# Attention, a mixer with an MLP, and a gated MLP on one core: weight splitting moved between engines and stages, and the element lists of the second product redrawn

## The chip, the cores and the metric

One core of one Trainium2 chip. The metric is the time of one execution on the device in microseconds; the median of the runs is used. Lower is better.

## What is computed

Three layers in a row, all in fp32, with batch 4, 576 positions and width 512.

```python
# attention: 8 heads of 64, window 128, a linear bias per head
scores = q @ k.T / 8 + bias;  attn = softmax(where(0 <= i - j < 128, scores, -1e9));  x = attn @ v
# "Moe": a mixer of rank 32 over positions, then an MLP 512 -> 2048 -> 512
u  = x + ((x.T @ U) @ V).T
x2 = u + maximum(u @ w_ch1, 0) @ w_ch2
# "Moe2": 512 -> 1024, half of it normalised and mixed over positions, a gate, and 512 -> 512
h = maximum(x2 @ w_in, 0);  a, v = h[..., :512], h[..., 512:]
v = w_spatial @ layernorm(v) + b_spatial
out = (a * v) @ w_out
```

## The kernel before

**Precision.** Every large fp32 product is done as three products of split numbers: each operand x is stored as a high part (a copy in the type fp32r) and a low part (x minus the high part, fp32r as well), and TensorE adds high x high, low x high and high x low in PSUM. So each operand needs a copy (in most places on ScalarE) and a subtraction (on VectorE or GpSimd).

**Seven products.** The two MLP products of Moe, `up` (512 -> 2048) and `down` (2048 -> 512), are each done in a block scheme in which seven half-sized products stand in for eight. It needs sums and differences of the four blocks of each operand (names A11, A12, A22, S1 to S4 on the side of the weights, m = 1 to 7 for the products).

**Stages on TensorE**, in order of time: attention with the mixer (16 pairs of heads; a step per pair, steps of the last batch overlap the start of `up`), `up` (24 units s = 0..23, that is 3 groups g of tokens by 8 pairs of columns u; a unit is 7 products of 6 matmuls of 384 columns), `down` (3 groups by 7 products by 8 entries kk of 6 matmuls of 384 columns), Moe2 (4 batches, each `half_v`, `half_u`, `spatial`, `output`).

**Order.** Each engine runs one instruction list written out by hand, with counting semaphores between them. All DMAs are issued by SyncE from one list. A wait in any list holds everything behind it in that list. The parts that matter here:

- In attention GpSimd makes the low parts of the attention output (`lo_x`, L656) and the split of the first unit of w_ch1 (`first_w1`, L691 to L703), and at its end sums and low parts of the first group of u (`x_sum`, `lo_xs`, L665 to L682). VectorE's reads of PSUM, scores (L1167), copies (L1176) and denominators (`sums`, L1183 to L1186) are steps of the same chain. SyncE loads q/k and v two pairs ahead at most (`load_qk`, `load_v`, L375 and L382).
- In `up` ScalarE keeps three partial results per unit (`keep_p`, L934), writes one block (`c21`), VectorE adds the others (`c11` L1368, `c12` L1374, `relu_b` L1380, `c22` L1386), and SyncE stores the four blocks of a unit to DRAM, r_scr (`store_r`, L421). The staging tile has two halves, so the additions of unit s wait for the store of unit s-2. `keep_p(s, 7)` must be done before the product (s, 4).
- w_ch2 is split during `up`, one of its 8 parts kk at a time, in the units that `W2_UNIT = {9: 0, 10: 1, 11: 2, 12: 3, 13: 4, 14: 5, 17: 6, 18: 7}` names: VectorE forms four sums (L1344 to L1349), ScalarE the high parts (`w2_shi_of` L925, `w2_hi_of` L918 and L919; L925 waits until all six stores of the part before have landed), VectorE the low parts (L1353, L1329, L1331), SyncE stores them (`store_w2`, L440 to L443, six DMAs) and they are read back in seven pieces of 2 MB (`load_w2q`, L447).
- In `down` the relu'd blocks a, b, c, d come back (`load_raw`, L451). `raw_c` lies in memory that `up` uses to its end. Each entry is one kk: ScalarE writes its high part (`hi_r`, L953), VectorE its low part (`lo_r`, L1393, L1396), in a ring of `RING = 5` tiles of 384 columns. Sums of blocks (`r_sum`, L1405, L1410, L1415, L1419) are made in halves of 1536 columns, and the list puts `r_sum(0, 3, 0)` right behind the fourth entry of the first product. `add_res` (L1429) and `dc` (L1439, L1446) add the residual and the partial results.
- Moe2's weights (17 parts: 4 of w_in's v half, 4 of its u half, 4 of w_out, 5 of w_spatial) are loaded into the four slots of `w1raw` (`load_wc`, L502 and L503) and split in the last group of `down` and behind it: ScalarE `hi_wc` (L982, L984), GpSimd `lo_wc` (L710). The high parts of the v half come behind entry 0 of product (2, 2), those of the u half together with `hi_x2` (L994) behind entry 1 of (2, 4), those of w_out in (2, 3), and those of w_spatial behind the last entry, in front of `relu_v(0)` (L1081), which frees the PSUM tile of `half_v` (L1805).

## Time and profile before

| | |
|---|---|
| median of 3 runs | 808.46 us (808.29 to 809.04) |
| the profiled execution | 811.25 us, span 809.5 us |
| attention until the first product of `up` | 0 to about 150 us of the span |
| `up` | to about 376 us |
| `down` | to 587.03 us |
| Moe2 | to the end |

The boundaries are read from the first and last matmuls of each part. Parts overlap a little: two tail steps of attention run among the first units of `up`. "Busy" counts a matmul from its start to its modelled end, and matmuls overlap; where the text counts matmuls in a stretch, the product of count and pace tells more than the busy time.

### The profile page before, as it was taken

The numbers are of one execution on the slowest core, as the hardware profiler recorded it, in microseconds if no ns is written. First come the engines' busy times: TensorE is split into PE (matmuls) and PEld (weight loads), VectorE is DVE, ScalarE is ACT, GpSimd is POOL, SyncE is SP. The second block draws the span as 40 slices with busy tenths as digits, with TensorE's granted clock in tenths as the row PEclk, the third lists the DMA queues.
The fourth block names the chain that finished last, engine by engine and source line by source line (L and its number), as shares of the span: only waits on it lengthen the run. The fifth ranks groups of instructions, "written<-read, shape, count | busy, mean of one in ns | idle before, by whom it ended". The sixth has DMA issues, their size and how long they took to land.

```text
span 809.5 us, 13413 instructions
## 1 busy us (share of the span) xinstructions
PE 739.8 (91%) x4688; PEld 678.3 (84%) x4688; DVE 491.4 (61%) x1149; ACT 377.8 (47%) x889; POOL 97.5 (12%) x77
## 2 busy tenths in 40 slices
PE   8999999889998788895589999979879999999998
PEld 5777777789997778894589989969869899899998
DVE  6877787877675566321586896795827436416422
ACT  5977787635443343322235455536535233342322
POOL 1611136700000000000000000121331010000100
PEclk9999999999999899898779999999999999999999
DMA  6433242345368876599855625623460010000101
GB/s 205 124 110 103 88 152 73 130 156 183 120 234 279 284 241 206 192 384 421 313 183 191 195 77 197 246 65 121 131 247 1 1 60 1 25 34 0 58 0 59
DMA packets 74547, 119.20 MB, mean 147 GB/s; under 512 B 4992, under 2 KB 56704, under 8 KB 73600
## 3 DMA queue, kind: packets, MB, share of 16 engines
q1 hardware_dynamic: 74496, 118.55, 42.7%
q8 instruction: 29, 0.48, 0.2%
q14 instruction: 22, 0.18, 0.1%
HBM read 70.82 MB, written 47.71 MB: 146 GB/s over the span
## 4 chain that ended last, share of the span: by engine, by line
PE 70%; DVE 10%; DMA 10%; issue 4%; SPq 3%; ACT 3%; POOL 0%; DVEq 0%; ACTq 0%
PE bank L1840 4%; PE bank L1841 4%; PE bank L1842 4%; PE bank L1682 4%; PE wide L1697 3%; PE bank L1878 3%; PE bank L1880 3%; PE bank L1879 3%; PE bank L1989 2%; PE bank L1664 2%; DMA w_scr<-tok 2%; PE bank L1991 2%; PE bank L1990 2%; PE bank L1807 2%; PE bank L1805 2%
## 5 line engine op out<-in xcount | busy, mean ns | idle before, releaser
L1840 PE MATMUL bank<-xs,w1s 128*128 128x384 f32 x336 | 118.7, 353 | 20.0 <-ACT sums_u L934 15.8
L953 ACT ACTIVATE rk<-tok 128x384 fp32r<-128x384 f32 x144 | 73.6, 525 | 97.5 <-PE wide L1880 48.7
L1841 PE MATMUL bank<-xs,w1s 128*128 128x384 f32 x336 | 116.7, 347 | 0.0
L1842 PE MATMUL bank<-xs,w1s 128*128 128x384 f32 x336 | 116.5, 347 | 0.0
L1878 PE MATMUL bank<-rk,w2q 128*128 128x384 f32 x208 | 73.1, 351 | 32.0 <-DVE rk L1393 28.3
L1840 PEld LDWEIGHTS bank<-xs,w1s 128*128 128x128 f32 x336 | 66.4, 198 | 24.4 <-ACT sums_u L934 18.3
L796 ACT ACTIVATE sc<-sc,mn 128x256 f32<-128x256 f32 (+1 forms) x144 | 67.0, 468 | 20.7 <-DVE mn L1167 20.6
L934 ACT ACTIVATE sums_u<-bank 128x384 f32<-128x384 f32 x72 | 35.2, 489 | 83.0 <-PE bank L1842 80.0
L1878 PEld LDWEIGHTS bank<-rk,w2q 128*128 128x128 f32 x208 | 40.2, 193 | 37.5 <-DVE rk L1393 30.5
L1880 PE MATMUL bank<-rk,w2q 128*128 128x384 f32 x208 | 71.1, 342 | 0.0
L1879 PE MATMUL bank<-rk,w2q 128*128 128x384 f32 x208 | 71.1, 342 | 0.0
L1841 PEld LDWEIGHTS bank<-xs,w1s 128*128 128x128 f32 x336 | 66.6, 198 | 0.0
L1842 PEld LDWEIGHTS bank<-xs,w1s 128*128 128x128 f32 x336 | 66.4, 198 | 0.0
L1396 DVE TENSOR_TENSOR rk<-tok,rk 128x384 fp32r<-128x384 f32 x96 | 51.0, 564 | 23.0 <-ACT rk L953 23.0
L710 POOL TENSOR_TENSOR wvl<-w1raw,wvh 128x512 fp32r<-128x512 f32 x4 | 7.5, 1896 | 362.8 <-ACT wvh L984 362.8
L1167 DVE CUSTOM_DVE_ANT_0 sc<-bank,bias 128x256 f32<-128x256 f32 (+1 forms) x128 | 42.3, 384 | 5.4 <-PE bank L1644 3.5
L1176 DVE COPY pt<-bank 128x512 f32<-128x512 f32 x48 | 31.4, 682 | 20.8 <-PE bank L1682 20.8
L1878 PE MATMUL wide<-rk,w2q 128*128 128x384 f32 x128 | 43.3, 338 | 0.6 <-DVE rk L1396 0.5
L1880 PE MATMUL wide<-rk,w2q 128*128 128x384 f32 x128 | 43.0, 336 | 0.0
L1879 PE MATMUL wide<-rk,w2q 128*128 128x384 f32 x128 | 43.0, 336 | 0.0
L1879 PEld LDWEIGHTS bank<-rk,w2q 128*128 128x128 f32 x208 | 40.3, 194 | 0.0
L1880 PEld LDWEIGHTS bank<-rk,w2q 128*128 128x128 f32 x208 | 40.2, 193 | 0.0
(222 smaller groups left out, 1830.7 us busy)
## 6 DMA issues: line engine op xcount, KB each, us to landing
r_scr<-tok SPq DMA_DIRECT2D x19, 768.0 KB, 4.1
w2q<-w_scr SPq DMA_DIRECT2D x7, 2048.0 KB, 14.5
tok<-r_scr SPq DMA_DIRECT2D x18, 768.0 KB, 5.8
qkraw<-qk SPq DMA_DIRECT2D x32, 288.0 KB, 3.0
w1raw<-w SPq DMA_DIRECT2D x32, 256.0 KB, 3.7
w_scr<-tok SPq DMA_DIRECT2D x12, 512.0 KB, 3.5
u_scr<-tok SPq DMA_DIRECT2D x6, 768.0 KB, 4.6
raw_c<-r_scr SPq DMA_DIRECT2D x6, 768.0 KB, 4.6
```

The lines of the kernel that those rows point to most:

```text
L796: act.activation(w, w, ACT.Exp, bias=mn[:, s, n:n + 1], scale=-1.0, accum_out=sm[:, i, c:c + 1]).then_inc(exp_done, 1)
L934: act.activation(sums_u[:, i, :], a_ps[s % 2][:, 0:HT], ACT.Copy).then_inc(kept, 1)
L953: act.activation(rk[:, n % RING, 0], raw[RAW_OF[m]][:, kk, :], ACT.Relu if m <= 3 else ACT.Copy).then_inc(rk_hi, 1)
L1167: dve.tensor_tensor_reduce(out=out, in0=src, in1=add, scale=-SCALE, scalar=3e38, op0=ALU.add, op1=ALU.min, accum_out=mn[:, s, n:n + 1]).th ...
L1396: dve.tensor_tensor(lo, x, hi, ALU.subtract).then_inc(rk_lo, 1)
L1682: last = pe.transpose(pt_ps[f % 2][:, j * P:(j + 1) * P], sc[:, i % 2, n, w * P:(w + 1) * P], ident[:, :])
L1840: pe.matmul(o, wh, ah, start=(k == 0 and m in FRESH), stop=False, skip_group_check=True)
L1841: pe.matmul(o, wl, ah, start=False, stop=False, skip_group_check=True)
L1842: last = pe.matmul(o, wh, al, start=False, stop=(k == 1), skip_group_check=True)
L1878: pe.matmul(o, wh, rh, start=(kk == 0 and m in FRESH), stop=False, skip_group_check=True)
L1879: pe.matmul(o, wl, rh, start=False, stop=False, skip_group_check=True)
L1880: last = pe.matmul(o, wh, rl, start=False, stop=(kk == UNITS - 1), skip_group_check=True)
```

## The change

It has four parts.

1. **Moe2's weights.** SyncE loads the 17 parts in attention into nine slots of a new tile `wprep` (at the place where `xs` lies later), GpSimd makes both the high part (`tensor_copy`) and the low part (in place), SyncE stores them to a new DRAM tensor `wc_scr`. The tables WC_AFTER, WC_LOAD and WC_STORE say at which pair. They are read back as finished pairs near the end of `down` (`load_group`), and `hi_wc`, `lo_wc` are gone. SyncE's and GpSimd's attention loops are unrolled.
2. **w_ch2.** The sums and the low parts are GpSimd's (`split_w2`), the high parts stay with ScalarE, later in the unit (behind `keep_p(s, 6)`), and wait for the stores of the six blocks' classes separately (`w2_out_t` for A11, A12, A22; `w2_out_s` for S1 to S4). W2_UNIT becomes 9, 10, 11, 12, 13, 15, 16, 18.
3. **`down`'s lists.** An entry is a pair of kk (768 columns), `RING` is 3 such entries, sums are made in quarters at places that FIRST_T and NEXT_T name, the last unit of `up` already makes the first three high parts, the loads are ordered anew, `raw_c`, `late`, `u_in` and the `w2q` tiles have other places.
4. **Small moves.** The low parts of m = 7, 5, 4 of the first group of u go from GpSimd to VectorE; the last four mixer products (`mix_up`) are spread over units 1 to 4 where three of them stood in unit 2; stores of u follow at unit 5.

```diff
-RING = 5
+RING = 3
+DP = UNITS // 2
+SLOTS = 9
-W2_UNIT = {9: 0, 10: 1, 11: 2, 12: 3, 13: 4, 14: 5, 17: 6, 18: 7}
+W2_UNIT = {9: 0, 10: 1, 11: 2, 12: 3, 13: 4, 15: 5, 16: 6, 18: 7}
+WC_AFTER = {0: [0, 1], 1: [2, 3], 2: [4], 3: [5, 6], 4: [7, 8, 9], 5: [10, 11, 12], 6: [13], 7: [14, 15, 16]}
+WC_LOAD = {3: [2, 3], 4: [4], 5: [5, 6], 6: [7, 8, 9], 7: [10, 11, 12], 8: [13], 9: [14, 15, 16]}
+WC_STORE = {3: [0, 1], 5: [2, 3], 6: [4], 7: [5, 6], 8: [7, 8, 9], 9: [10, 11, 12], 10: [13], 12: [14, 15, 16]}
+FIRST_T = {(2, 2): [(3, 0)], (2, 3): [(3, 1), (2, 0)], (6, 0): [(2, 1), (4, 0)], (6, 1): [(3, 2), (2, 2)],
+           (6, 2): [(3, 3), (2, 3)], (6, 3): [(1, 0), (4, 1)], (5, 0): [(1, 1), (4, 2)],
+           (5, 1): [(1, 2), (4, 3)], (5, 2): [(1, 3)]}
...
+            def store_wc(m):
+                w = DM if m < WS else S
+                sp.wait_ge(wc_ready, m + 1)
+                sp.dma_start(wc_scr[m, :, :, 0:w], wprep[:, m % SLOTS, :, 0:w]).then_inc(wc_out[m % SLOTS], 16)
...
+            for p in range(PAIRS, (B - 1) * PAIRS):
+                load_qk(*divmod(p, PAIRS))
+                load_v(*divmod(p - 1, PAIRS))
+                prepare(p)
...
                 if s in W2_UNIT:
                     kk = W2_UNIT[s]
-                    if kk >= 1 and kk + 1 < UNITS:
-                        load_w2(kk + 1)
                     store_w2(kk)
+                    if kk + 2 < UNITS:
+                        load_w2(kk + 2)
                 if s == LATE + 1:
...
-                    for n in "abd":
+                    for n in "ab":
                         load_raw(0, n, 0)
                         load_raw(0, n, 1)
...
+                if s == LATE + 2:
+                    load_raw(0, "d", 0)
+                    load_raw(0, "d", 1)
-            sp.wait_ge(up_p, UP_AT[(NU - 2, 3)])
-            load_w2q(5)
             sp.wait_ge(up_p, UP_AT[(NU - 1, 3)])
+            sp.wait_ge(r_out[0], 16 * NU // 2)
             load_raw(0, "c", 0)
             load_raw(0, "c", 1)
             store_r(NU - 1)
-            load_w2q(7)
-            load_w2q(4)
+            load_w2q(5)
...
+            def split_wc(m):
...
+                pool.tensor_copy(hi, x).then_inc(wc_hi, 1)
+                pool.wait_ge(wc_hi, m + 1)
+                pool.tensor_tensor(x.bitcast(F32R), x, hi, ALU.subtract).then_inc(wc_ready, 1)
...
+            def split_w2(kk):
...
+                pool.tensor_tensor(s[:, 0], ra[:, QP:2 * QP], rb[:, QP:2 * QP], ALU.add).then_inc(w2_sum, 1)
+                pool.tensor_tensor(s[:, 2], ra[:, 0:QP], ra[:, QP:2 * QP], ALU.subtract).then_inc(w2_sum, 1)
+                pool.tensor_tensor(s[:, 1], s[:, 0], ra[:, 0:QP], ALU.subtract).then_inc(w2_sum, 1)
+                pool.tensor_tensor(s[:, 3], rb[:, 0:QP], s[:, 1], ALU.subtract).then_inc(w2_sum, 1)
+                pool.wait_ge(w2_hi, 3 * kk + 1)
+                pool.tensor_tensor(ra[:, 0:QP].bitcast(F32R), ra[:, 0:QP], w2_top[0].bitcast(F32R), ...)
+                pool.wait_ge(w2_hi, 3 * kk + 2)
+                pool.tensor_tensor(pair.bitcast(F32R), pair, w2_top[1].bitcast(F32R), ...)
+                pool.wait_ge(w2_hi, 3 * kk + 3)
+                for h in range(2):
+                    two = s[:, 2 * h:2 * h + 2]
+                    pool.tensor_tensor(two.bitcast(F32R), two, w2_top[2][:, 2 * h:2 * h + 2].bitcast(F32R), ...)
...
                 keep_p(s, 6)
...
+                if s in W2_UNIT:
+                    w2_hi_of(W2_UNIT[s])
+                    w2_shi_of(W2_UNIT[s])
                 if u == 0:
                     hi_xs(g, 3)
+                if s == NU - 1:
+                    for n in range(RING):
+                        hi_r(n)
                 keep_p(s, 7)
...
-                if g == G - 1 and kk == 1 and m == 4:
-                    for c in range(WU, WO):
-                        hi_wc(c)
+                if g == G - 1 and j == 0 and m == 3:
+                    act.wait_ge(rk_used, DN_AT[(G - 1, 6)])
                     hi_x2(0, [0, 1, 2])
```

## Rows read from the trace of the kernel before

**Rows 1.** The page: busy time of each engine, share of the span, instructions.
```profile
PE 739.8 (91%) x4688; PEld 678.3 (84%) x4688; DVE 491.4 (61%) x1149; ACT 377.8 (47%) x889; POOL 97.5 (12%) x77
```
**Rows 2.** Stretches of `up`: start:end length, busy (count) per engine, clock, DMA, GB/s.
```profile
341.02:348.30 7.28, 7.28 (x44) 7.28 (x43) 2.04 (x4) 1.97 (x4) 0.00 (x0) 1.00 0.85 283
174.03:187.73 13.70, 11.30 (x59) 10.93 (x58) 8.77 (x20) 3.92 (x8) 0.00 (x0) 0.88 0.29 98
232.63:333.74 101.11, 83.54 (x422) 80.69 (x421) 56.03 (x104) 38.41 (x71) 0.00 (x0) 0.90 0.75 253
239.91:283.58 43.67, 35.03 (x172) 33.75 (x171) 22.14 (x44) 14.94 (x28) 0.00 (x0) 0.88 0.86 286
```
**Rows 3.** Stretches of `down` and of the start of Moe2, same columns.
```profile
355.00:375.00 20.00, 16.67 (x95) 16.05 (x94) 5.74 (x12) 6.33 (x14) 0.00 (x0) 1.00 1.03 424
375.00:420.00 45.00, 25.75 (x121) 24.75 (x120) 26.29 (x36) 11.11 (x22) 0.00 (x0) 0.73 0.75 299
465.00:480.00 15.00, 13.72 (x75) 12.47 (x74) 14.83 (x21) 6.98 (x14) 0.00 (x0) 1.00 0.24 80
520.00:545.00 25.00, 18.91 (x99) 16.40 (x98) 23.13 (x26) 10.46 (x21) 7.47 (x4) 1.00 0.31 108
565.00:587.00 22.00, 17.77 (x99) 16.70 (x98) 16.44 (x25) 12.08 (x25) 9.66 (x7) 1.00 0.46 132
592.00:605.00 13.00, 8.84 (x32) 6.79 (x32) 2.14 (x4) 4.54 (x8) 6.05 (x5) 0.87 0.76 258
```
**Rows 4.** Waits: who waited for what, total us, times, longest us.
```profile
ACT tok L925 <- DMA w_scr<-tok: 20.3, 4, 6.6
...
DVE tok L1405 <- DMA raw_c<-r_scr: 15.8, 1, 15.8
...
DVE sums_d L1429 <- DMA u_in<-u_scr: 6.4, 1, 6.4
...
PE wide L1805 <- ACT vr L1081: 4.2, 1, 4.2
```
**Rows 5.** GpSimd's operations by shape: count, busy us, mean ns, idle before.
```profile
L703 POOL TENSOR_TENSOR w1s<-wst,w1s 128x1024 fp32r<-128x1024 f32 x1 | 2.4, 2373 | 5.8 <-ACT w1s L882 5.8
...
L698 POOL TENSOR_TENSOR w1s<-w1raw,w1s 128x512 fp32r<-128x512 f32 x1 | 1.3, 1282 | 0.0
...
L694 POOL TENSOR_TENSOR wst<-wst,w1raw 128x256 f32<-128x256 f32 x1 | 0.7, 734 | 0.0
```
**Rows 6.** Steps of attention, same columns as rows 2 (fifth busy time is GpSimd).
```profile
69.61:78.14 8.53, 8.53 (x76) 6.25 (x76) 6.79 (x29) 6.56 (x22) 1.56 (x1) 1.00 0.34 107
...
125.66:134.29 8.63, 8.61 (x76) 6.25 (x76) 7.49 (x30) 7.13 (x24) 4.75 (x3) 1.00 0.00 1
```
**Rows 7.** Timeline: a VectorE operation beside GpSimd's, start, us, operation; then GpSimd's own.
```profile
24.45 0.43 DVE L1183 TENSOR_SCALAR den<-sm 128x9 f32<-128x9 f32 x1
...
150.79 2.06 DVE L1301 TENSOR_TENSOR wst<-w1raw 128x256 f32<-128x256 f32 x1
...
148.74 5.80 POOL L682 TENSOR_TENSOR xs<-tok,xs 128x768 fp32r<-128x768 f32 x3
```
**Rows 8.** DMA of 225 to 335 us: GB/s in 40 slices; issues with KB each, us to landing.
```profile
GB/s 145 159 0 237 310 334 344 206 298 340 298 228 230 336 349 214 279 342 147 285 355 334 350 210 263 341 176 174 3 252 34 0 268 353 383 251 181 64 336 267
...
w_scr<-tok SPq DMA_DIRECT2D x12, 512.0 KB, 3.5
...
w_scr<-w1raw SPq DMA_DIRECT2D x8, 256.0 KB, 3.4
```
**Rows 9.** VectorE and ScalarE by shape: `lo_r`, `r_sum`, `lo_xs` (VectorE), `w2_shi_of` (ScalarE).
```profile
L1396 DVE TENSOR_TENSOR rk<-tok,rk 128x384 fp32r<-128x384 f32 x56 | 29.5, 554 | 13.7 <-ACT rk L953 13.7
...
L1405 DVE SCALAR_TENSOR_TENSOR tok<-raw_c,tok 128x1536 f32<-128x1536 f32 x3 | 5.2, 1749 | 0.0
...
L1271 DVE TENSOR_TENSOR xs<-tok,xs 128x768 fp32r<-128x768 f32 x7 | 6.6, 952 | 2.9 <-ACT xs L869 2.9
...
L925 ACT ACTIVATE tok<-wst 128x1024 fp32r<-128x1024 f32 x4 | 4.2, 1056 | 20.3 <-DMA w_scr<-tok 20.3
```

More of the change, by code:

```diff
@@ L402, in _, with load_wc, prepare @@
                 sp.dma_start(mvraw[r * RANK:(r + 1) * RANK, :], mv).then_inc(mix_in, 16)
+            def load_wc(m):
+                slot = m % SLOTS
+                if m >= SLOTS:
+                    sp.wait_ge(wc_out[slot], 16 * (m // SLOTS))
+                if m < WU:
+                    src = w_in[1, m]
+                elif m < WO:
+                    src = w_in[0, m - WU]
+                elif m < WS:
+                    src = w_out[(m - WO) * P:(m - WO + 1) * P, :]
+                else:
+                    t = m - WS
+                    src = w_sp[t * P:t * P + rows(t), :]
+                    if t == TILES - 1:
+                        sp.dma_start(wprep[TAIL:P, slot, 1, :], src).then_inc(weights_in[slot], 16)
+                        sp.dma_start(wprep[0:TAIL, slot, 1, :], src).then_inc(weights_in[slot], 16)
+                        return
+                sp.dma_start(wprep[:, slot, 1, 0:DM if m < WS else S], src).then_inc(weights_in[slot], 16)
+            def store_wc(m):
+                w = DM if m < WS else S
+                sp.wait_ge(wc_ready, m + 1)
+                sp.dma_start(wc_scr[m, :, :, 0:w], wprep[:, m % SLOTS, :, 0:w]).then_inc(wc_out[m % SLOTS], 16)
+            def prepare(p):
+                for m in WC_STORE.get(p, []):
+                    store_wc(m)
+                for m in WC_LOAD.get(p, []):
+                    load_wc(m)
+            load_wc(0)
+            load_wc(1)
             load_qk(0, 2)
@@ L406, in _ @@
             load_v(0, 2)
+            prepare(3)
             load_w1(1)
@@ L744, in _ @@
             pool.tensor_tensor(mvl[:, :], mvraw[:, :], mvh[:, :], ALU.subtract).then_inc(mix_ready, 1)
+            for m in WC_AFTER[0]:
+                split_wc(m)
             lo_x(0, 0)
             first_w1()
-            lo_x(0, 1)
-            with pool.Fori(1, B - 1) as b:
-                for i in range(PAIRS):
-                    lo_x(*((b, i - 2) if i >= 2 else (b - 1, i + 2)))
+            for p in range(1, (B - 2) * PAIRS + 2):
+                lo_x(*divmod(p, PAIRS))
+                for m in WC_AFTER.get(p, []):
+                    split_wc(m)
             lo_x(B - 2, 2)
@@ L999, in _ @@
             step(B - 1, 0)
+            for slot in range(SLOTS):
+                act.wait_ge(wc_out[slot], wc_total(slot))
             hi_xs(0, 1)
```

438 lines of the change are left out of this document (187 added, 251 removed).

## Prediction

> **What bounds the kernel now.** First the page's busy line: TensorE 91% of the span, every other engine far below [rows 1]. So the time is TensorE's work plus the places where it waits, and the waits table and the stretches are read next. An undisturbed unit of `up` takes 7.28 us for 42 matmuls, 0.173 us each, at clock 1.00 [rows 2]. Against this pace each stretch has a loss: its length less its count times 0.173. The ten units around the w_ch2 split take 101.11 us instead of 72.8: 28.3 lost. Inside them, four units take 43.67 (10.9 each) with DMA 86% busy. The unit with three mixer products takes 13.70, of which 16 matmuls of 288 columns at 0.13 (the pace by columns) are 2.1: 4.3 lost [rows 2]. In `down`: 355 to 375 loses 3.6 (95 matmuls are 16.4), 375 to 420 loses 24 (121 are 20.9), 465 to 480 2.0, 520 to 545 7.9, 565 to 587 4.9. At 592 to 605, 32 matmuls of 512 columns at 0.231 (again by columns) are 7.4 of 13: 5.6 lost [rows 3]. The waits name the reasons: VectorE 15.8 us for raw_c and 6.4 for u_in, ScalarE 20.3 for the stores of w_ch2 parts, TensorE 4.2 for the relu of v, which stands behind the w_spatial copies [rows 4]. Together these losses are some 80 us. The change addresses nearly all of them.
>
> **Part 1, Moe2's weights.** *Attention.* Added on GpSimd: 17 x (copy + subtraction). The subtraction of 512 columns is 1.28 us; the copy is not in the trace, its bounds are 0.73 (256 columns) and 2.37 (1024), and I take 1.28, the row of its width [rows 5]. So 2.6 per part, 44 us in all. Pairs 4 to 7 carry 10 parts: 26 us and 4 x 1.56 of `lo_x` in some 34 us of steps [rows 6]. It fits, as a low part is needed two steps later. GpSimd does disturb VectorE: an addition of 256 columns beside the three `lo_xs` took 2.06 us, one GpSimd operation's length (5.80 / 3) [rows 7]. In attention VectorE's main work reads PSUM; only the three tiny `sums` operations do not (one took 0.43 [rows 7]). Two steps compare: 1.56 us of GpSimd gives 8.53, 4.75 gives 8.63 [rows 6]. So 0.1 per 3.2 us, for 44 us 1.4. The ends are 0 and 8 steps x 3 operations x 1.3 = 31; I take 1.4, as the steps are the same work. The Trainium skill (SBUF — State Buffer, "Who interferes with whom") calls this an exclusive lock for a whole instruction, for VectorE operations with two SBUF inputs or in a two-port mode. By that rule only the `sums` operations can wait here, and the term would be the same 0 to 31. The rows agree as far as they go.
>
> SyncE's list: a store of parts waits for GpSimd with the next q/k load behind it. The tightest is pair 4: stores of parts 0 and 1, two loads and w_ch1 stand in front, 2.1 MB, 6 us at some 340 GB/s (the fastest slices of [rows 8] are 334 to 355), plus the load itself 2, against one step of lead. I take +1; ends 0 and +8 (one for each batch of stores). Below nothing is excluded for both, since attention loses no work. Part 1 here: **+2.5**.
>
> *End of `down` and Moe2's start.* ScalarE's four copies per group (about 2 us in the list before `hi_r`) and GpSimd's beside them go. The stretch 520 to 545 has them and the burst of half sums; I leave 2.5 of 7.9 (block d must still come back from DRAM just before its use): **-5.5**. The stretch 565 to 587 keeps one wait of 1.1 for `keep_dp` and half a us at the end: **-3**. The relu of v no longer stands behind w_spatial's copies: **-5.5** of 5.6. w_spatial now lands about 9 us after the last entry (2.95 MB at 340), needed 25 us after it (`half_v` 56 x 0.231 and `half_u` 96 x 0.13). If the cover were gone, it would cost the 9.
>
> **Part 2, w_ch2.** Per part GpSimd needs 4 x 0.73 + 0.73 + 1.28 + 2 x 1.28 = 7.5 us [rows 5], just over a unit. The loop over the sums' stores: high part 1.06 [rows 9], low parts 2.56, issues 1.0, landing 3.5 [rows 8] = 8.1. The loop over the blocks' stores: copies 1.0, low part 1.3, issues and the last landing (3.4) about 5 = 7.4. And the bytes: 1792 KB of stores, 768 of r_scr, 512 of w_ch2 are 3.15 MB; at 340 GB/s 9.25 us. So I expect DMA to pace: 9.5 us for each of units 10 to 13, 2.2 lost in each. ScalarE, where `w2_shi_of` waits, has `keep_p(s, 7)` queued behind it, and TensorE's (s, 4) behind that: such a wait becomes TensorE's at once, less about 1 us of slack (so unit 9 loses 0.5). Units 15 and 16 get parts together with the second exchange of `xs`: GpSimd's operations delay the `lo_xs` (0.95 [rows 9]) by up to one operation each, and ScalarE has 2.9 us of work between `keep_p` 6 and 7 where 2 fit: 3 lost. Unit 18: 0.5. Sum 13 instead of 28.3: **-15**. Ends: at the 8.1 loop -22; at today's 10.9 per unit -8.
>
> The Trainium skill (GPSIMD Engine Reference, "Engine selection") says to leave elementwise work of two inputs to VectorE, since GpSimd takes about twice as long. The trace agrees: 1.93 us for 768 columns [rows 7] against 0.95 [rows 9]. By it GpSimd would pace the loop at 7.5 us or more, and DMA at 9.25 still ends last, so the sum stays.
>
> **Part 3, `down`'s lists.** *Units 22 and 23*: the stores of `late` stand behind two fewer raw loads (1.5 MB): -2.5, against +0.5 for three `hi_r` of 768 columns in front of `keep_p(23, 7)`: **-2** of 3.6. *Start of `down`*: raw_c no longer stands behind w2q 5 (2 MB, 4.9 us at the 424 GB/s of [rows 3]), and it is first asked for behind entry 6, so 12.5 us (6 x 12 x 0.173) after the start. Late next is VectorE itself: eight entries carry two quarter sums each (a half took 1.75), 3 x 0.95 = 2.85 us [rows 9] against 2.08 on TensorE, so 6 lost, plus 1 for `dc`, less the ring's lead: 6. u_in stands behind one w2q instead of two: 2 at most, under the lead. One us for the clock, which was at 0.73 in this stretch after 12 us of idle and hardly falls now. So 8 of 24 stay: **-16**; ends -8 (raw_c still late) and -20. *Group 1* (465 to 480): sums are spread over 11 entries, 11 x 0.95 + 16 x 0.95 + 3 = 28.6 against 22.9, less lead 3.5: 2.5 instead of 2.0: **+0.5**, ends -2 and +4. A `lo_r` of two kk costs 0.95 instead of 2 x 0.554 [rows 9]; VectorE saves 4 us a group, in the sum already.
>
> **Part 4, small moves.** `mix_up` spread: TensorE no longer waits for add after add; the last one still waits some 2: **-2.5** of 4.3. Three `lo_xs` moved to VectorE: 2.9 us there instead of 5.8 on GpSimd, with which VectorE's w_ch1 sums collided (2.06 each [rows 7]): **-1**, ends -3 and +1.
>
> **Sum**: 2.5 - 5.5 - 3 - 5.5 - 15 - 2 - 16 + 0.5 - 2.5 - 1 = -47.5. The profiled execution took 811.25 (span 809.5), 2.8 over the median; from its time 763.75, on the median 808.46 - 47.5 = **761**.
>
> **Rivals.**
> 1. *Forecast*, 748 to 773: chance 0.68.
> 2. *The split of w_ch2 stays as slow as now.* GpSimd's 7.5 us is just over a unit, each operation beside VectorE's may wait, and ScalarE now waits for GpSimd's sums with `keep_p` behind it. For it: 1.93 against 0.95 for the same width. Against: GpSimd has nothing else then, and 7.5 is far from 10.9. Without the 15: 776. Chance 0.14. The Trainium skill (GPSIMD Engine Reference, "Engine selection") points this way.
> 3. *The start of `down` and attention give back half*: raw_c is not earlier, since 13 MB (loads of 3, 2, 1.5, 2, 2 and three stores of 0.8) are queued from unit 20 on, 31 us at 424 GB/s, and q/k loads stand behind stores of parts. 761 + 8 + 6 = 775, both with the second 785. Chance 0.12.
> 4. *Slower*: GpSimd's lock holds attention's chain for each added operation: 34 x 1.28 = 44, and in `up` the 15 are not won: 761 + 44 + 15 = 820. It decides from 47 us on. Against it stand the two equal steps [rows 6]. Chance 0.04. The Trainium skill's lock (SBUF — State Buffer, "Who interferes with whom") would do this if the reads of PSUM took it too.
> 5. *No effect of the lists*: each wait is replaced by the next and a few us remain: 800. Chance 0.02.
>
> **Numbers.** 0.2% is 1.6 us, about what a measurement of this kernel can tell from no change. Range: the forecast's own 748 to 773 and upward to the second and third rivals, 786; the fourth and most of the fifth are outside. Faster 0.95, same 0.01, slower 0.04.
>
> **What would show it.** Steps of attention at 8.5 to 8.7 and no wait of TensorE for qkraw but near pair 4; units 10 to 13 at about 9.5 us with DMA above 90%; ScalarE's longest wait there on w_scr stores, not on GpSimd; no idle over 3 us between `up` and `down`, small waits for VectorE's rk in products 6 and 5 of group 0; no wait before the third tile of `half_v`. It would be wrong if attention's steps grew by over 1 us where GpSimd splits, if ScalarE waited for GpSimd's sums, or if raw_c still landed late.

## The result and the profile after

The changed kernel takes 778.1 us (median of four runs, 776.17 to 779.41) beside 808.75 for the kernel before: a ratio of 0.9616, interval 0.9590 to 0.9642. In a second set of runs it took 775.85 us beside 810.32, ratio 0.9588 (0.9569 to 0.9606). So it is faster by 3.8 to 4.1%, some 31 to 34 us. The forecast was 761, so 17 us of the forecast gain are missing in the medians, and the experiments look for them. The profiled execution took 776.17 us, with a span of 774.3.

Its page, engine busy time and the DMA total:

```profile
PE 728.7 (94%) x4688; PEld 670.6 (87%) x4688; DVE 454.5 (59%) x1036; ACT 352.6 (46%) x788; POOL 161.8 (21%) x155
...
DMA packets 82514, 137.68 MB, mean 178 GB/s; under 512 B 5536, under 2 KB 57248, under 8 KB 81568
```

VectorE has 113 instructions fewer than in [rows 1], GpSimd 64 us more work, TensorE the same 4688 matmuls at 94% of a shorter span. That says that waits went, not where. For that the same events are looked up in both traces (`relu_b(s)` is VectorE's relu at the end of unit s of `up`, `keep_dp(g, 7)` ScalarE's copy of product 7 in group g of `down`), and the time from one to the next is compared with the terms of the forecast. All times are of the two profiled executions.

| from - to | before | after | change | forecast |
|---|---|---|---|---|
| start - `relu_b(0)` | 166.57 | 165.90 | -0.7 | +1.5 |
| `relu_b(0)` - `relu_b(8)`, with `mix_up` | 66.06 | 64.71 | -1.4 | -2.5 |
| `relu_b(8)` - `relu_b(18)`, split of w_ch2 | 101.11 | 90.14 | -11.0 | -15 |
| `relu_b(18)` - `relu_b(21)` | 21.84 | 21.85 | 0 | 0 |
| `relu_b(21)` - `keep_dp(0, 7)`, start of `down` | 82.67 | 77.53 | **-5.1** | **-18** |
| `keep_dp(0, 7)` - `keep_dp(1, 7)` | 68.96 | 68.33 | -0.6 | +0.5 |
| `keep_dp(1, 7)` - last product of `down` | 79.82 | 69.41 | -10.4 | -8.5 |
| Moe2 and output | 222.47 | 216.43 | -6.0 | -5.5 |
| span | 809.5 | 774.3 | -35.2 | -47.5 |

The missing 12.3 us are made of 12.9 at the start of `down`, 4.0 in the split, 1.1 at `mix_up`, less 5.7 by which the other terms came out better. The spans of the two profiled executions lie 35.2 us apart and the medians 30.7, since the one before is 2.5 us above its median and the one after 1.9 below; these some 4.5 us belong to no term.

The stretches in the windows view of the kernel after (start:end length, busy and count of TensorE, weight load, VectorE, ScalarE, GpSimd, then granted clock, DMA share, GB/s): two steps of attention, unit 4, the split, its units 10 to 13, the start of `down`:

```profile
69.61:78.14 8.53, 8.53 (x76) 6.24 (x76) 6.86 (x29) 6.55 (x22) 6.87 (x6) 1.00 1.00 345
125.66:134.29 8.63, 8.61 (x76) 6.25 (x76) 7.49 (x30) 7.13 (x24) 4.74 (x3) 1.00 0.01 2
189.21:200.29 11.08, 8.72 (x51) 8.33 (x50) 6.99 (x15) 3.64 (x7) 0.00 (x0) 1.00 0.20 71
230.61:320.75 90.14, 77.75 (x422) 75.22 (x421) 35.58 (x51) 38.44 (x71) 61.76 (x60) 0.96 0.81 273
237.89:276.73 38.84, 32.73 (x170) 31.77 (x169) 8.60 (x17) 14.63 (x28) 29.66 (x33) 0.91 0.97 325
342.60:420.13 77.53, 60.77 (x317) 58.04 (x316) 41.66 (x53) 22.85 (x33) 0.00 (x0) 0.91 0.84 324
```

**Attention** is untouched. Its first two rows are the steps of [rows 6], at the same start to 0.01 us and of the same length, although GpSimd's busy time in the first rose from 1.56 to 6.87 us and DMA from 0.34 to 1.00. So the 0.1 us between the two steps, which the forecast put down to GpSimd's 1.56 against 4.75 us, was not GpSimd's. **The split**: units 10 to 13 take 9.7 us each with DMA 0.97 busy (0.86 before [rows 2]); the forecast had 9.5, paced by DMA. **The start of `down`**: 16.8 of 77.53 us without TensorE's busy time, at clock 0.91. The timeline of the kernel after shows where (start, duration, engine, line, operation, and in brackets the idle time before it and what ended it):

```profile
342.98 0.94 SPq L480 DMA_DIRECT2D r_scr<-late  x1
...
355.91 0.56 DVE L1385 TENSOR_TENSOR late<-bank,sums_u 128x384 f32<-128x384 f32 x1 [5.67 <-DMA r_scr<-late]
...
357.94 0.41 PE L1886 MATMUL bank<-rk,w2q 128*128 128x384 f32 x1 [4.53 <-DVE rk L1410]
...
367.10 0.39 SPq L480 DMA_DIRECT2D r_scr<-late  x1
367.53 1.11 SPq L507 DMA_DIRECT2D w2q<-w_scr  x1
...
376.27 0.89 SPq L536 DMA_DIRECT2D u_in<-u_scr  x2
...
382.21 1.03 DVE L1443 TENSOR_TENSOR sums_d<-sums_d,u_in 128x384 f32<-128x384 f32 x2 [8.43 <-DMA u_in<-u_scr]
...
384.16 0.69 PE L1886 MATMUL bank<-rk,w2q 128*128 128x384 f32 x1 [7.64 <-DVE rk L1410]
```

Two stops, 4.53 and 7.64 us, each behind one VectorE instruction that waits for DMA. The first, `c11(23)` (L1385), writes to the half of `late` that unit 21 left, and the store of unit 21, issued at 342.98, has landed only when it starts at 355.91. The second, `add_res(0, 11)` (L1443), waits for u_in. SyncE issues that load at 376.27 only, since it waits for the last unit's store, issued at 367.10. The load then shares the DMA engines with the weight load of 367.53, and 5.9 us go by till the addition. `lo_r` stands behind the addition, and TensorE behind `lo_r`. Then the clock:

```profile
375.00:380.00 5.00, 1.51 (x9) 1.19 (x7) 0.00 (x0) 0.00 (x0) 0.00 (x0) 0.90 0.96 396
380.00:385.00 5.00, 0.84 (x3) 0.84 (x4) 2.79 (x5) 0.00 (x0) 0.00 (x0) 0.50 1.07 440
385.00:390.00 5.00, 5.00 (x19) 4.97 (x18) 3.92 (x5) 1.69 (x2) 0.00 (x0) 0.58 1.02 436
```

After the idle 7.64 us the granted clock is 0.58, not far above the lower level (1.2 of 2.4 GHz): in the last row TensorE is busy for all 5 us and does 19 matmuls where 29 fit.

### The profile page after: what moved, and what is told of

The parts are those of the page before. It is cut to its first block, busy times and chain, and to the rows that moved or that the text cites. A ratio compares the mean times of both kernels' runs of the same rounds, so it can differ in the third digit from the quotient of the medians.

```text
span 774.3 us, 13225 instructions
## 1 busy us (share of the span) xinstructions
PE 728.7 (94%) x4688; PEld 670.6 (87%) x4688; DVE 454.5 (59%) x1036; ACT 352.6 (46%) x788; POOL 161.8 (21%) x155
## 4 chain that ended last, share of the span: by engine, by line
PE 73%; DVE 12%; DMA 5%; issue 4%; POOL 3%; ACT 2%; SPq 1%; DVEq 0%; ACTq 0%; POOLq 0%
PE bank L1847 5%; PE bank L1849 5%; PE bank L1848 5%; PE bank L1689 4%; PE wide L1704 3%; DMA r_scr<-late 3%; PE bank L1886 3%; PE bank L1888 3%; PE bank L1887 3%; PE bank L1995 2%; PE bank L1671 2%; PE bank L1997 2%; PE bank L1996 2%; PE bank L1814 2%; PE bank L1812 2%
## 5 line engine op out<-in xcount | busy, mean ns | idle before, releaser
L1847 PE MATMUL bank<-xs,w1s 128*128 128x384 f32 x336 | 115.8, 345 | 13.4 <-ACT sums_u L1012 8.1
L1848 PE MATMUL bank<-xs,w1s 128*128 128x384 f32 x336 | 114.2, 340 | 0.0
L1849 PE MATMUL bank<-xs,w1s 128*128 128x384 f32 x336 | 114.1, 340 | 0.0
L1029 ACT ACTIVATE rk<-tok 128x768 fp32r<-128x768 f32 x72 | 60.6, 847 | 92.2 <-PE wide L1888 30.8
L859 POOL TENSOR_TENSOR vl<-vr,vh 128x512 fp32r<-128x512 f32 x8 | 11.3, 1407 | 398.0 <-ACT vh L1156 398.0
L1847 PEld LDWEIGHTS bank<-xs,w1s 128*128 128x128 f32 x336 | 64.6, 192 | 17.0 <-ACT sums_u L1012 10.2
L1848 PEld LDWEIGHTS bank<-xs,w1s 128*128 128x128 f32 x336 | 64.7, 192 | 0.0
L1849 PEld LDWEIGHTS bank<-xs,w1s 128*128 128x128 f32 x336 | 64.5, 192 | 0.0
L1413 DVE TENSOR_TENSOR rk<-tok,rk 128x768 fp32r<-128x768 f32 x48 | 45.4, 953 | 24.5 <-ACT rk L1029 24.0
```

The lines of the kernel that those rows point to most:

```text
L1029: act.activation(rk[:, n % RING, 0], raw[RAW_OF[m]][:, 2 * j:2 * j + 2, :], ACT.Relu if m <= 3 else ACT.Copy).then_inc(rk_hi, 1)
L1413: dve.tensor_tensor(lo, x, hi, ALU.subtract).then_inc(rk_lo, 1)
L1847: pe.matmul(o, wh, ah, start=(k == 0 and m in FRESH), stop=False, skip_group_check=True)
L1848: pe.matmul(o, wl, ah, start=False, stop=False, skip_group_check=True)
L1849: last = pe.matmul(o, wh, al, start=False, stop=(k == 1), skip_group_check=True)
```

## The experiments

Eleven further kernels ran, and the changed kernel once more. A line number is that of the run's own kernel, which can lie a few lines from the changed kernel's. A profile gives one execution of each; the stretch named in the text is read from it. Unit s is the time from `relu_b(s-1)` to `relu_b(s)`, as in the prediction; the expectations of the runs with half the stores and with the copy of the sums count the units 10 to 13 one lower.

**The residual's addition later.**

```
-                    if m in (1, 6, 7):
-                        add_res(g, {1: 11, 6: 12, 7: 22}[m])
+                    if m in (6, 7) or (m == 1 and g):
+                        add_res(g, {1: 11, 6: 12, 7: 22}[m])
...
                     if m == 2:
+                        if g == 0:
+                            add_res(0, 11)
                         dc(g, 11)
```

> VectorE's first add of the residual in the down half, which waited 8.4 us for the load of u_in, moves behind three more entries, to just before dc(0,11) (line 1453's first call). The theory that this wait is what the missing 13 us at the start of the down half are made of: TensorE's gap of 7.64 us before 384.16 goes, and with it part of the 2 to 3 us that a granted clock of 0.5 to 0.6 cost after it; the copy of product (0,7), at 420.13 us in the changed kernel, comes 6 to 10 us earlier, the kernel runs in 768 to 772 us. Its rival, that VectorE's list of quarter sums paces these 60 us anyway (two sums per entry): the gap is only spread over the entries, the copy of (0,7) comes at most 2 us earlier, the kernel stays at 776 to 778 us.

Measured: 770.71 us, ratio 0.9523 (0.947 to 0.9576). The whole stretch, and its middle, in the windows view:

```profile
341.91:410.76 68.85, 59.98 (x317) 57.32 (x316) 41.47 (x53) 22.84 (x33) 0.00 (x0) 0.95 0.92 365
375.00:380.00 5.00, 5.00 (x29) 4.63 (x27) 3.92 (x5) 1.69 (x2) 0.00 (x0) 1.00 0.96 394
380.00:385.00 5.00, 2.46 (x13) 2.04 (x12) 4.97 (x9) 0.84 (x1) 0.00 (x0) 1.00 1.07 441
```

77.53 became 68.85 us, 8.7 less, for the same instructions (317 matmuls, 53 VectorE operations). (The changed kernel's second profile and the six runs below that leave this stretch alone have 76.8 to 78.7.) So the wait for u_in was two thirds of the missing 12.9 us, and the rival, VectorE's pace, falls as the main cause. It is what comes next: from 380 to 385 VectorE is 4.97 of 5 us busy and TensorE 2.46.

**The load of raw b behind two weight blocks**, on top of it: in SyncE's list the loads of b go from unit 20 to unit 23.

```
                 if s == LATE + 1:
...
-                    for n in "ab":
-                        load_raw(0, n, 0)
-                        load_raw(0, n, 1)
+                    load_raw(0, "a", 0)
+                    load_raw(0, "a", 1)
...
+                if s == NU - 1:
+                    load_raw(0, "b", 0)
+                    load_raw(0, "b", 1)
```

> On top of the late add_res (770.7 us) SyncE issues the loads of raw b, 1.6 MB, in unit 23 instead of in unit 20, where they stand ahead of the store of unit 21 that VectorE's c11(23) waits for (it lands 12.5 us after its issue). The theory that this store is late because of the bytes issued before it: it lands some 3.7 us earlier, TensorE's gap of 4.5 us before 357.2 shrinks to under 1 us, and with it goes the granted clock of 0.78; the copy of product (0,7) stands 4 to 6 us earlier against relu_b(22), the kernel runs in 765 to 767 us. Its rival, that the store shares the engines with what is issued after it (second weight, d): it lands less than 1 us earlier, or b then lands too late for VectorE's first quarter sum (372 us), and the time stays at 770 to 772 us.

Measured: 767.68 us, ratio 0.9483 (0.9459 to 0.9507).

```profile
343.38 0.34 SPq L480 DMA_DIRECT2D r_scr<-late  x1
...
353.48 0.56 DVE L1387 TENSOR_TENSOR late<-bank,sums_u 128x384 f32<-128x384 f32 x1 [2.85 <-DMA r_scr<-late]
...
356.49 0.41 PE L1890 MATMUL bank<-rk,w2q 128*128 128x384 f32 x1 [2.68 <-DVE rk L1412]
...
371.47 0.96 DVE L1424 SCALAR_TENSOR_TENSOR tok<-raw_c,tok 128x768 f32<-128x768 f32 x1 [1.58 <-DMA raw_c<-r_scr]
```

The store lands by 353.5, 10.1 us after its issue instead of 12.9, and TensorE's stop is 2.68 instead of 4.53. So what is issued ahead of a store did delay this one, by 2.8 us where 3.7 were expected. VectorE now waits 1.58 us for raw_c, which stands behind the moved load, and the stretch wins 1.7 us net (67.11), less than half of the 4 to 6 expected. Two of the combinations below, which have both edits, repeat it (67.06 and 67.16). The intervals of the two ratios overlap, so the times alone do not show the gain.

**`mix_up`'s last call later**: in TensorE's list from behind (4, 2) to behind (4, 5), its addition behind `c22(4)`.

```
-                elif (s, m) == (4, 2):
+                elif (s, m) == (4, 5):
                     mix_up(B - 1, 3, bank[6:8])
...
-                for k in {2: [0], 3: [1], 4: [2, 3]}.get(s, []):
+                for k in {2: [0], 3: [1], 4: [2]}.get(s, []):
...
                 c22(s)
+                if s == 4:
+                    add_u(B - 1, 3, bank[6:8])
```

> The last of mix_up's four calls moves in TensorE's order from behind (4,2) to behind (4,5), and VectorE's add for it from before c22(4) to behind it. The theory that unit 4 takes 11.08 instead of 7.28 us because TensorE waits (2.36 us) for the add of the call before, which is queued behind c11(4) and the low parts: unit 4's period falls to 8 to 9.5 us (the call itself takes 1.3 of it), relu_b(18) at 320.75 us comes 2 to 3 us earlier, the kernel runs in 775 to 776 us. Its rival, that the wait is the work that VectorE has in this unit: the period stays above 10.5 us and the time at 778 us.

Measured: 774.27 us, ratio 0.9557 (0.9506 to 0.9608). The row of the changed kernel, then that of this one:

```profile
192.52 0.40 PE L1758 MATMUL wide<-mvh,tst 128*128 128x288 f32 x1 [2.36 <-DVE tok L1265]
```

```profile
196.27 0.40 PE L1760 MATMUL wide<-mvh,tst 128*128 128x288 f32 x1 [0.27 <-DVE tok L1265]
```

The wait is gone and unit 4 takes 9.14 us; the changed kernel's own two profiles have 11.08 and 11.11. That is 2.0 us, and sometimes more: five other runs with the same unit 4 have 12.5 to 12.7 us, the wait of 2.36 the same and the granted clock 0.86 or 0.87 instead of 1.00. The profiled execution lost 1.8 to 2.3 us in unit 1, ahead of any edit, and so did the combination of all edits below; the two other combinations did not (7.18 and 7.21 us), and why is not known. So the stretch shows the cause, and the median (774.27, below the 775 to 776 expected) cannot confirm it.

**The second weight in units 14 and 17 instead of 15 and 16.**

```
-W2_UNIT = {9: 0, 10: 1, 11: 2, 12: 3, 13: 4, 15: 5, 16: 6, 18: 7}
+W2_UNIT = {9: 0, 10: 1, 11: 2, 12: 3, 13: 4, 14: 5, 17: 6, 18: 7}
```

> Two of the eight calls that split the second weight move: from units 15 and 16 to units 14 and 17, as before the change; GpSimd, ScalarE and SyncE follow the same table. The theory that units 15 and 16 lose 6.5 us (10.87 and 10.22 against 7.28) because GpSimd's subtractions and VectorE's x operations hold each other up: units 15 and 16 fall back to 7.3 to 8 us, unit 14 becomes DMA-paced like 10 to 13 (9 to 9.7 us), unit 17 takes at most 8.5; the kernel runs in 774 to 776 us. Its rival, that the stores and loads of this stretch pace it wherever they are put: as much is lost in units 14 and 17 as is won in 15 and 16, and the time stays within 1 us of 778.

Measured: 773.48 us, ratio 0.9544 (0.9492 to 0.9595). Units 14, 16 and 18:

```profile
276.56:287.14 10.58, 8.79 (x51) 8.37 (x49) 4.29 (x6) 5.09 (x9) 9.02 (x9) 1.00 0.99 329
295.31:302.78 7.47, 7.32 (x43) 7.03 (x42) 4.59 (x7) 3.00 (x6) 0.00 (x0) 1.00 0.29 105
310.06:318.84 8.78, 7.56 (x44) 7.24 (x43) 2.12 (x4) 3.63 (x7) 6.99 (x8) 1.00 0.94 323
```

Units 15 and 16 fall from 21.1 us together to 15.6, but unit 14 rises from 8.4 to 10.6 and unit 18 from 7.3 to 8.8, both with DMA at 0.94 to 0.99. From `relu_b(8)` to `relu_b(18)` it is 86.57 us, beside 90.14 and 88.24 in the changed kernel's two profiles: 1.7 to 3.6 less; four other runs with the calls in their old units have 87.5 to 88.3, so about 1 to 2 less. Of the 5.5 us won in units 15 and 16, most comes back where the calls now stand.

**The second weight's sums and low parts on VectorE** (`split_w2` cut in two: `w2_sum_of` behind `relu_b(s - 1)`, `w2_low_of` behind `c22(s)`).

```
-            for kk in range(UNITS):
-                split_w2(kk)
...
                 relu_b(s - 1)
+                if s in W2_UNIT:
+                    w2_sum_of(W2_UNIT[s])
...
                 c22(s)
+                if s in W2_UNIT:
+                    w2_low_of(W2_UNIT[s])
```

> The sums and low parts of the second weight run on VectorE instead of GpSimd, 8 operations of 256 to 512 columns a unit, some 4 us; the order of lists, transfers and ScalarE's copies stays that of the changed kernel. The theory that units 10 to 13 are paced by the DMA engines (0.97 busy, 325 GB/s): their period stays 9.5 to 9.9 us; units 15 and 16 lose less or more than 6.5 us as VectorE's own 4 us count or the lock does; the kernel runs in 776 to 782 us. Its rival, that GpSimd's chain of sums and subtractions (1.28 us a piece) paces them: the period falls below 9 us and the kernel below 775 us. A third, that VectorE had no room for it, which is what the change bought: the period rises to 11 us or more and the kernel runs in over 785 us.

Measured: 782.06 us, ratio 0.9669 (0.9612 to 0.9726). Units 10 to 13:

```profile
239.31:281.42 42.11, 33.48 (x170) 32.21 (x169) 21.86 (x48) 14.73 (x28) 0.00 (x0) 0.92 0.91 300
```

GpSimd's chain did not pace these units: without it they take 10.5 us instead of 9.7. Nor was VectorE full (21.86 of 42.11 us). The parts are ready later, since they stand behind `c22`: SyncE, whose stores wait for the low parts, waited 16.5 us for them in these units against 6.7 in the changed kernel, and DMA is less busy (0.91). Units 15 and 16 take 20.9 us, about as before, with no GpSimd operation there to hold VectorE up, but with the sums' own work added to VectorE's. So this run does not tell whether in the changed kernel the two engines hold each other up there; the next one does.

**Half the stores.** The low halves are not stored, and the loads of `down` read the high half twice, so the product lacks its low part and counts the high one again.

```
-                for h, a11, rest in ((0, w2_top[0], w2_top[1]),
-                                     (1, ra[:, 0:QP], rb.rearrange("p (q c) -> p q c", c=QP))):
+                for h, a11, rest in ((0, w2_top[0], w2_top[1]),):
...
-                for h, four in ((0, w2_top[2]), (1, w2_sums(kk))):
+                for h, four in ((0, w2_top[2]),):
```

> The changed kernel without the stores of the second weight's low halves (half of the store's bytes, 0.92 MB a call; the loads of the down half read the high half twice, so the low part is left out of the product, with the same number of multiplications). GpSimd, ScalarE and VectorE do all that they did. The theory that bytes pace units 9 to 13: 3.1 MB a unit become 2.2 MB, 6.5 us at 340 GB/s, less than TensorE's 7.28; the units fall from 9.2 (12.2 in unit 11) to 7.3 to 7.8 us, relu_b(14) comes 8 to 10 us earlier, the kernel runs in 764 to 769 us. Its rival, that GpSimd's chain (7.3 to 7.8 busy of 9.2 us) or ScalarE's order paces them: the period stays above 8.5 us, the kernel runs in over 773 us.

Measured: 769.64 us, just above the 764 to 769 expected, ratio 0.9487 (0.9464 to 0.951).

```profile
238.37:267.99 29.62, 29.62 (x170) 29.06 (x169) 8.83 (x16) 14.94 (x28) 29.31 (x33) 1.00 0.90 301
```

Units 10 to 13 take 7.4 us each with TensorE busy throughout, while GpSimd does all its work (29.31 of 29.62 us). `relu_b(14)` comes 8.7 us earlier than in the changed kernel's first profile, 6.5 earlier than in its second. So the stores pace these units. Their number falls with their bytes, from six a call to three, and this run does not separate the two. GpSimd at 99% busy is no bound yet, but there is no room left on it either.

Units 15 and 16 keep their loss: 10.48 and 10.25 us, where the changed kernel's profiles have 10.5 to 10.9 and 10.2. So halving the stores wins nothing there. In unit 16 the profile puts ScalarE's wait in front of the copy of the sums down to a store, and the store, 4.6 us from its issue at 295.11, does land then; but GpSimd's fourth sum ends at the same time, and with half the stores the wait is as long and is put down to that sum. TensorE's stop in this unit, for VectorE's low part of x, is the same 2.41 us in both. The changed kernel, then this run:

```profile
297.87 0.41 PE L1847 MATMUL bank<-xs,w1s 128*128 128x384 f32 x1 [2.41 <-DVE xs L1320]
298.39 1.34 POOL L781 TENSOR_TENSOR tok<-w1raw,tok 128x256 f32<-128x256 f32 x1
...
299.82 1.06 ACT L1003 ACTIVATE tok<-tok 128x1024 fp32r<-128x1024 f32 x1 [2.48 <-DMA w_scr<-wst]
```

```profile
288.74 0.41 PE L1848 MATMUL bank<-xs,w1s 128*128 128x384 f32 x1 [2.41 <-DVE xs L1321]
...
290.70 1.06 ACT L1004 ACTIVATE tok<-tok 128x1024 fp32r<-128x1024 f32 x1 [2.48 <-POOL tok L782]
```

GpSimd's four sums of 256 columns take 0.9 to 1.44 us each there, beside VectorE's x operations, and 0.74 mostly in units 10 to 13; VectorE's low parts of x take up to 2.05 instead of 0.95. The two engines stretch each other, and the sums, the copy and the low parts come late by it.

**The copy of the sums behind `keep_p(s, 7)`.**

```
                     w2_hi_of(W2_UNIT[s])
-                    w2_shi_of(W2_UNIT[s])
...
                 keep_p(s, 7)
+                if s in W2_UNIT:
+                    w2_shi_of(W2_UNIT[s])
```

> One call on ScalarE moves: the copy of the four sums' high parts (line 1003, which waits 1.9 us for the stores of the call before) goes from before keep_p(s,7) to behind it. In units 9 to 12 of the changed kernel TensorE stops once a unit, for 1.65 us, and for just that copy of a product. The theory that the DMA engines pace these units (1.01 to 1.04 busy, some 3.1 MB a unit at 335 to 348 GB/s, 9.2 us): the stop goes, and another takes its place (a copy or a sum that waits for its store or its load), since the bytes stay the same; units 9 to 12 keep 9.2 us a unit and the kernel stays within 1.5 us of 778. Its rival, that it is ScalarE's order and not the bytes: each of the four units falls to 7.4 to 8 us, and with the stops goes the granted clock of 0.77 in unit 11; relu_b(18) comes 6 to 9 us earlier, the kernel runs in 769 to 773 us.

Measured: 774.58 us, ratio 0.9558 (0.9527 to 0.9588). The changed kernel first, unit 11: ScalarE's copy waits for a store, the copy of the product behind it is late, and TensorE stops.

```profile
251.84 1.06 ACT L1003 ACTIVATE tok<-tok 128x1024 fp32r<-128x1024 f32 x1 [1.94 <-DMA w_scr<-wst]
252.80 0.85 ACT L1012 ACTIVATE sums_u<-bank 128x384 f32<-128x384 f32 x2
...
253.33 0.44 PE L1847 MATMUL bank<-xs,w1s 128*128 128x384 f32 x1 [1.66 <-ACT sums_u L1012]
```

With the copy moved, unit 10 and then units 11 to 13, and unit 15:

```profile
239.27:246.55 7.28, 7.28 (x44) 7.28 (x43) 2.14 (x5) 3.58 (x7) 5.88 (x8) 1.00 0.88 288
246.55:273.66 27.11, 23.30 (x128) 21.70 (x127) 6.61 (x13) 10.05 (x20) 21.32 (x24) 1.00 1.02 338
282.44:295.10 12.66, 7.65 (x36) 7.08 (x35) 10.69 (x11) 6.83 (x12) 10.08 (x7) 0.76 0.79 272
```

Unit 10 is free of loss. The other three take 9.0 us each at DMA 1.02, and TensorE stops for `keep_p` again, 0.92 to 1.05 us at a time, behind other copies that wait for stores. The time lies outside both ranges, and both readings held half: the order decides who stops and when (34.4 us instead of 36.6 to 38.8 for the four units in the seven profiles above and below that have these units as in the changed kernel), the DMA engines at 1.02 keep the three units at 9.0 us. Unit 15 takes 2 us more than in the changed kernel and unit 16 2 less.

**More work on GpSimd in attention.**

```
-                pool.tensor_copy(hi, x).then_inc(wc_hi, 1)
-                pool.wait_ge(wc_hi, m + 1)
+                for n in range(2):
+                    pool.tensor_tensor(hi, x, x, ALU.add).then_inc(wc_hi, 1)
+                    pool.wait_ge(wc_hi, 3 * m + n + 1)
+                pool.tensor_copy(hi, x).then_inc(wc_hi, 1)
+                pool.wait_ge(wc_hi, 3 * m + 3)
```

> In attention GpSimd gets, for each of the 17 weight pieces, two further additions of 128x512 elements whose result is overwritten: 34 operations of some 1.27 us, 43 us. The forecast put 2.5 us on attention for 32 us of such work and the trace showed none. The theory that GpSimd's work in attention delays VectorE as long as they overlap, only that VectorE has slack for it: the steps of attention (8.53 and 8.63 us) now grow by 0.1 to 0.4 us and the down half starts 1 to 5 us later, 779 to 783 us. A rival, that GpSimd itself is then the chain (its own low parts of x come behind the pieces): steps grow by over 1 us and the kernel runs in over 790 us. A third, that attention is untouched by anything on GpSimd up to its capacity: the same step starts to 0.05 us, 776 to 779 us.

Measured: 791.23 us, ratio 0.9769 (0.9745 to 0.9793). `relu_b(0)` comes at 183.15, 17.3 us later. Two stretches of 20 us, and the longest of TensorE's waits in the first 160:

```profile
20.00:40.00 20.00, 14.57 (x132) 10.78 (x130) 12.56 (x52) 15.11 (x48) 19.48 (x20) 0.93 0.51 172
...
80.00:100.00 20.00, 13.15 (x115) 9.39 (x115) 12.04 (x46) 11.10 (x38) 19.11 (x19) 0.88 0.71 233
```

```profile
PE wide L1747 <- POOL xl L699: 7.3, 1, 7.3
PE bank L1654 <- DMA qkraw<-qk: 5.4, 1, 5.4
```

This is the second of the three theories, GpSimd as the chain: in the stretches with 19.5 and 19.1 of 20 us TensorE waits for the q/k loads, which stand in SyncE's list behind the stores of parts, and for its low part of x. The two waits are 12.7 of the 17.3 us, and the clock in these stretches fell to 0.93 and 0.88. (Between 40 and 80 us GpSimd has 19.1 and 18.7 of 20, and TensorE no such wait.) The changed kernel's busiest stretches, from 20 to 80 us, have 14.4 to 16.5 of 20 us and no such wait. So it left some 20% of GpSimd free at the tightest place.

**All five edits together.**

> The five single edits together: add_res late, raw b late, mix_up late, the copy of the sums behind keep_p(s,7), second weight in units 9 to 14, 17 and 18. If each keeps what its stretch showed (8.7 us at the start of the down half, 3.4 before product (0,1), 3.5 in unit 4, 1 for units 14 and 17, 2 to 4 for the copy), the kernel runs in 757 to 762 us. The theory of bytes says that the last two don't add, since they move waits within a stretch with the same bytes: 761 to 765 us.

Measured: 761.29 us, ratio 0.9378 (0.9356 to 0.9399). The start of `down` from `relu_b(22)` is 59.88 us, but `relu_b(8)` to `relu_b(18)` is 85.77, hardly below the 86.57 of the moved units alone and the 86.03 of the moved copy alone. The two edits of the split do not add.

**With the second weight's calls spread**:

```
-W2_UNIT = {9: 0, 10: 1, 11: 2, 12: 3, 13: 4, 14: 5, 17: 6, 18: 7}
+W2_UNIT = {9: 0, 10: 1, 12: 2, 13: 3, 14: 4, 17: 5, 18: 6, 19: 7}
```

> As the run with all edits, but the second weight's calls stand in units 9, 10, 12, 13, 14, 17, 18 and 19: gaps in which the DMA engines catch up. The theory of bytes: 11 units of 7.28 us give 80 us, and the stretch moves 27 MB, 80 us at 340 GB/s, so nearly all of the 11 us that units 9 to 18 still lose can go, 4 to 8 us against the run with all edits. Its rival, that the stores of unit 19 delay the loads of raw a, d and the first weight block, which wait for them: what is won is lost before product (0,1) or (0,2), and the time stays within 2 us of the run with all edits.

Measured: 760.53 us, ratio 0.9374 (0.9353 to 0.9395).

```profile
235.07:264.19 29.12, 29.12 (x170) 29.12 (x169) 8.77 (x17) 12.86 (x25) 20.88 (x24) 1.00 0.94 316
264.19:277.34 13.15, 9.29 (x51) 8.33 (x49) 5.91 (x6) 5.09 (x9) 10.51 (x11) 1.00 1.00 339
...
337.44:401.96 64.52, 53.34 (x275) 49.90 (x274) 39.55 (x49) 20.86 (x29) 0.00 (x0) 0.92 0.98 380
```

With unit 11 left free, units 10 to 13 lose nothing, DMA at 0.94. `relu_b(8)` to `relu_b(18)` is 79.74 us, 6.0 less, though one of the eight calls now stands behind this stretch. But unit 14 takes 13.15, and the start of `down` 4.6 more than in the run with all edits (TensorE's stop for the store of unit 21 is 4.82 us there, 2.68 in that run). The rival held: the end is the same within 1 us.

**Spread, none in unit 19**, and in unit 14 the copy of the sums ahead of `keep_p` again (units 9, 10, 12, 13, 14, 16, 17, 18).

> As the spread run, with two changes: the second weight's calls stand in units 9, 10, 12, 13, 14, 16, 17 and 18, so that none delays the loads of raw a in unit 20; and in unit 14 alone the copy of the sums stands before keep_p again, since behind it, it held up the copies of x and unit 14 lost 5.9 to 6.5 us instead of 3.3. If both readings hold: unit 14 takes 10 to 11 us, units 16 to 18 together lose 3 to 4, relu_b(18) comes within 2 us of the spread run's 79.7 us behind relu_b(8), the start of the down half is that of the run with all edits (59.9 us from relu_b(22) to the copy of product (0,7), against 64.5); the kernel runs in 755 to 759 us. If the bytes decide wherever the calls stand: what unit 11's and 15's holes save is lost in units 16 to 18, and the time is 760 to 762 us.

Measured: 759.34 us, ratio 0.939 (0.9365 to 0.9415), between the two ranges. The start of `down` is 59.8 us, as forecast, but `relu_b(8)` to `relu_b(18)` is 85.33, back at the 85.77 of the run with all edits. Unit 14 is worse, not better:

```profile
273.21 1.06 ACT L1005 ACTIVATE tok<-tok 128x1024 fp32r<-128x1024 f32 x1 [3.31 <-DMA w_scr<-wst]
...
274.69 0.69 PE L1856 MATMUL bank<-xs,w1s 128*128 128x384 f32 x1 [5.28 <-ACT sums_u L1014]
```

It takes 15.42 us, and unit 18 takes 10.94. The copy waits for a store on either side of `keep_p`, 2.92 us in the spread run and 3.31 here, and ahead of `keep_p` it holds TensorE for 5.28 us. So the reading of unit 14 was wrong: its calls are behind their stores in either order, and this order costs 2.3 us more. The three combinations cannot be told apart by their intervals. Each is 50 to 51 us faster than the kernel before, and this one 16.5 faster than the changed kernel in the same set of runs.

**The changed kernel again.**

> The changed kernel once more, beside the last combination on the same chip: 776 to 779 us; its profile shows which of the readings above repeat (unit 1, unit 4, the 12.2 us of unit 11) and which were of one execution only.

Measured: 775.85 us, ratio 0.9588 (0.9569 to 0.9606). Unit 12 takes 9.73 us at clock 1.00 where the first profile had 12.22 at 0.77, so these 2.5 us of the first were of one execution. In the runs above that leave the order of units 10 to 13 alone, unit 12 takes 9.3 to 11.3 us, at clocks of 1.00 down to 0.85. From `relu_b(8)` to `relu_b(18)` the first profile has 90.14 us, the second 88.24 and four runs with the split unchanged 87.5 to 88.3, so the first is on the slow side. The start of `down` repeats: 77.9 us with stops of 4.98 and 6.75.

## Why the prediction was right, and where it was wrong

The direction held, and the time lies in the stated range of 748 to 786. But the forecast's own 748 to 773 was missed: 778.1 lies where the second and third rivals stood, and that it falls in the range is in good part luck, since it got there by the second's mechanism not at all and by the third's only in part. The split did win (-11.0 of 15, against "stays as slow as now"). In the third, raw_c was in time and attention lost nothing, though the start of `down` did give back more than its 8 us, and the queue of loads and stores that this rival named is behind the first of the two stops there. (Its "both with the second 785" adds up to 790 by its own terms.) The order of the terms did not hold either: the largest one, the start of `down` with units 22 and 23, came fourth.

- **Attention, +2.5**: 0. The copy took 0.61 us where the row of its width gave 1.28, so GpSimd had 32 us more instead of 44. The two nearly equal steps pointed the right way, though their 0.1 us was not GpSimd's. The terms for the lock and for SyncE's list were both covered; the run with more work shows where the cover ends.
- **The split, -15**: -11.0, or about -13 by the profiles of the four other runs with the same split (87.5 to 88.3 us). Pace and cause of units 10 to 13 were right (9.5 forecast; 9.7 and 9.3 in the two profiles), and the run with half the stores shows it. Units 15 and 16 lose 6.5 us, not 3. The step had the mechanism and was too small: GpSimd's and VectorE's operations held each other up, but it counted only VectorE's low parts as delayed. GpSimd's sums were late too, and in unit 16 ScalarE's copy waited 2.48 us for them with the copies of x behind it. That wait was one of the forecast's own signs of being wrong. The 0.5 us each for units 9 and 18 did not come (both 7.28).
- **Start of `down` with units 22 and 23, -18**: -5.1. The step that failed is "u_in stands behind one w2q instead of two: 2 at most, under the lead". The load's place in line was judged, not what it waits for before it is issued, which is the store of the last unit, and that landed 9 us after its issue. Nor was it seen that its reader stands in VectorE's list ahead of all `lo_r` of the next product. Moving that reader gives 8.7 us back, the 7.64 of the stop and one for the clock. The second failure is in "the stores of `late` stand behind two fewer raw loads": the stop of 4.53 us for the store of unit 21 stayed, and raw a and b are still ahead of it. The burst of quarter sums seems sized about right, though no run tests it alone: with the residual's addition late, the stretch of 68.85 us loses 14.0 against 0.173 a matmul, 9.5 of it beside the first stop (4.50 there), and the forecast left 9.6 of its 27.6. The forecast's signs had "no idle over 3 us between `up` and `down`"; both stops broke that.
- **`mix_up`, -2.5 of 4.3**: -1.4. The wait for the last addition was 2.36, as forecast ("some 2"), but unit 4 takes 3.8 us more than an undisturbed one (5.3 to 5.4 in the five runs with the lower clock), 2.8 of it beyond the call's own 8 matmuls of 0.13.
- **End of `down` (-8.5), group 1 (+0.5), Moe2 (-5.5), the first units (-1)**: -10.4, -0.6, -6.0, -0.7. Each within 2 us; the two residues left for the end of `down` were too large.

## What to carry to other kernels

For a transfer that is moved in a list, ask three things: what it waits for before it is issued, what is queued ahead of it, and what stands behind its first reader on that reader's engine. Only the second was asked here for u_in, and the other two cost 8.7 us. Where a stretch was paced by its stores, moving instructions mostly chose who waits; fewer stores, or a gap in which the queue empties, shortened it, and that gap must not push the loads of the next stage. And where two things release a wait at nearly the same time, the one that the profile names can be the wrong one to remove: taking the store away left ScalarE's 2.48 us in unit 16 as they were.
